# Spreading the slots' hidden inputs of six experts through a DRAM scratch tensor instead of TensorE products

## The chip, the cores and the metric

The kernel runs on one core of one Trainium2 chip. The metric is device time in microseconds (us), the median of several runs of the whole program. The engines are TensorE (PE, with its weight loads PEld), VectorE (DVE), ScalarE (ACT), GpSimd (POOL) and SyncE (SP, which here only issues DMAs).

## What is computed

Three layers in a row, in float32: an attention with a few global and some local keys (2 x 8 heads, 768 tokens, width 64), a soft mixture of experts over 32 slots, and a second mixture in which each of 1536 tokens goes to two of 8 experts. Cut to what matters here:

```python
# second layer; x is the soft layer's output, x = c @ slot_out: 32 slots' outputs mixed by the weights c
for e in range(E):                       # E = 8
    for k in range(2):
        mask = top2[:, k] == e
        h = np.maximum(x[mask] @ w1[e], 0.0)             # w1: 512 x 1024
        out[mask] += top2_w[mask, k, None] * (h @ w2[e]) # w2: 1024 x 512
```

The soft layer ends in a product with only 32 rows in the middle, so `x @ w1[e]` equals `c @ (slot_out @ w1[e])`. The kernel never makes x. It makes `g = slot_out @ w1[e]`, 32 x 1024, once for each expert, and then one product `c @ g` for each tile of 128 tokens.

## The kernel before, in words

The second layer is the stretch from 190 us to the end. Its work goes in tiles of 128 token rows, sorted by expert; each expert has at least two, here three or four, 28 in all. `run_tiles` calls `period(i, e, first, last)` for every tile i of every expert e, on each engine, with a first period, a loop over the middle ones and a last one. Each engine works through its own list in order.

A period on TensorE is: `down(0, i, e)`, twelve products of 512 columns with the first half of w2; `hidden` twice, eight products of 128 columns that make the next tile's h from `g_stack` (in the last period of an expert they read the next expert's part of it, and `wait_stack(e + 1)` stands before them); a transpose of a later tile's mixing weights; `down(1, i, e)`, twelve products with the second half. In the first period of an expert two things are added for the expert that follows, if `starts` says so (experts 2 to 7; experts 0 and 1 are made ahead of the loop): `slots_up(e + 1)` (line 1515) at its start makes g in bank 6, 128 partitions x 256 columns (four groups of 32 slots, one for each quarter of the 1024 columns), and `spread_slots_up(e + 1)` (line 1527) at its end lays it out as `g_stack` needs it.

g is kept as a sum of two float32r parts. ScalarE copies the high part to `g_hi` (`slots_up_high`), VectorE subtracts and stores the rest in `g_lo` (`slots_up_low`). `g_stack[:, e, :]` has 128 partitions x 1024: partitions 0 to 63 hold the high part twice, 64 to 127 the low part twice, and `c4T` holds the mixing weights split in the same way, so that one product over 128 partitions gives all the terms. Before the change eight products with the selection matrix `spread` (line 1538) put the parts in place in banks 2 and 3; ScalarE copies bank 2 and VectorE bank 3 to `g_stack` (`slots_up_spread`, lines 820 and 1141).

ScalarE also evacuates h (`hidden_high`, line 860) and the finished tile (`store_y`, line 880), and splits the next expert's w2 (`split_high`); VectorE makes the low parts (`hidden_low`, line 1224, `split_low`, line 1134). GpSimd fetches the mixing weights of a tile (line 667) and adds the stored tile to the output by an indirect DMA (line 695); it waits for the addition before it, and `store_y` waits for the addition of the tile two before, since `y_sb` has two buffers.

SyncE loads the weights, 2 MB for each of w1 and w2 of an expert, into a ring of four places, each from the fifth unit of this layer on in two halves of 1 MB with a wait for the first half before the second is issued. Its list `order` gives w1 and w2 by turns. Before it loads w1 of expert e + 2 it waits until `slots_up(e)` has used the place (`g_ready`), before w2 of e + 2 until w2 of e is split (`w_lo_stored`), and before w1 of expert 4 also until three tiles have been added to the output (`sums_before`, `out_added`).

Of the kernel before, what the change touches and what calls it, by code (L numbers as in the profile page):

```python
# [5 lines left out]
F32 = mybir.dt.float32  # L6
# [11 lines left out]
def attention_two_moe_layers(nc, q, k, v, n_global, n_local, phi, a_w1, a_w2,  # L18
# [52 lines left out]
    with ExitStack() as ctx:  # L71
# [214 lines left out]
        def sems(text):  # L286
            return [sem(n) for n in text.split()]
# [38 lines left out]
        tiles_ready, ids_made, hot_ready, slots_routed, tables_ready, rows_written = sems(  # L326
            "tiles_ready ids_made hot_ready slots_routed tables_ready rows_written")

        g_ready, g_hi_stored, g_lo_stored, g_spread, g_stored_act, g_stored_vec = sems(
            "g_ready g_hi_stored g_lo_stored g_spread g_stored_act g_stored_vec")  # L330
        w_hi_stored, w_lo_stored, w_rest_ready = sems("w_hi_stored w_lo_stored w_rest_ready")
        fetch_known, c_arrived, c4_ready, c4T_ready, c4T_stored = sems("fetch_known c_arrived c4_ready c4T_ready c4T_stored")
        first_arrived = [sem(f"first_arrived{n}") for n in range(FIRST)]
# [49 lines left out]

        ZERO_AFTER = (PAIRS - 1, NPAIR - 4)
        slot_rows = nc.dram_tensor("slot_rows", (N, ROW), F32).ap()
        block = ctx.enter_context(nc.Block())

        def path(eng):
# [41 lines left out]
        @block.sync  # L430
        def _(sp):
            def load_qk(p):
                b, hp = divmod(p, PAIRS)
                for n, t in enumerate((q, k)):
                    for h in range(2):
                        sp.dma_start(raw_qk[p % 2][n][:, :, h * HD:(h + 1) * HD],
                                     t[b, 2 * hp + h].rearrange("(i p) d -> p i d", p=P)).then_inc(qk_loaded[p % 2], 16)

            def load_v(p):
                b, hp = divmod(p, PAIRS)  # L440
                sp.dma_start(v_own[p % 2].rearrange("p h i d -> p (h i) d"),
                             v[b, 2 * hp:2 * hp + 2].rearrange("h (i p) d -> p (h i) d", p=P)).then_inc(v_loaded[p % 2], 16)

            def load_unit(n):
                layer, which, e = units[n]
                to, of = weights(units[n]), W[layer, which][e].rearrange("(c p) f -> p c f", p=P)
                chunks = to.shape[1] // halves(n)
                for h in range(halves(n)):
                    if h:

                        sp.wait_ge(unit_loaded[slot_of(n)], loaded(n) - 16)
                    own = slice(h * chunks, (h + 1) * chunks)
                    sp.dma_start(to[:, own], of[:, own]).then_inc(unit_loaded[slot_of(n)], 16)

            load_qk(0)
            load_qk(1)
            load_v(0)
            load_v(1)

            UNIT_AFTER = [p for p in range(-1, NPAIR - 2) if p != PAIRS - 1]  # L460
            assert len(UNIT_AFTER) == EARLY
            for p in range(-1, NPAIR - 2):
                if p + 3 < NPAIR:

                    sp.wait_ge(qk_transposed, 3 * (p + 2))
                    load_qk(p + 3)
                if p >= 0:

                    sp.wait_ge(heads_ready, QB * (p + 1))
                    load_v(p + 2)  # L470
                if p in UNIT_AFTER:
                    load_unit(UNIT_AFTER.index(p))
                if p in ZERO_AFTER:

                    sp.wait_ge(zeros_made, 1)
                    part = ZERO_AFTER.index(p)
                    first, end = [TT * n // len(ZERO_AFTER) for n in (part, part + 1)]
                    sp.dma_start(out.rearrange("(n p) d -> p n d", p=P)[:, first:end, :],
                                 zero_row[:].unsqueeze(1).to_broadcast([P, end - first, DM])).then_inc(rows_zeroed, 16)
                if p < 0:  # L480
                    sp.dma_start(phi_sb[:], phi.rearrange("(c p) s -> p c s", p=P)).then_inc(small_loaded, 16)
                    sp.dma_start(gate_sb[:, :, 0:E], w_gate.rearrange("(c p) e -> p c e", p=P)).then_inc(small_loaded, 16)
                    sp.dma_start(gate_sb[:, :, E:2 * E], w_noise.rearrange("(c p) e -> p c e", p=P)).then_inc(small_loaded, 16)

                    for t in range(TPG):
                        sp.dma_start(noise_sb[:, t * NG:(t + 1) * NG, :],
                                     noise.rearrange("(g t p) e -> t p g e", t=TPG, p=P)[t]).then_inc(small_loaded, 16)

            sp.wait_ge(heads_ready, UPB * B - QB)
            sp.wait_ge(qk_transposed, 3 * NPAIR)  # L490


            down1, up2, down2, up3, down3, up4 = range(2 * E + RING2 - 1, 2 * E + RING2 + 5)
            order = [*range(EARLY, down1), up2, down1, up3, down2, *range(down3, 4 * E)]
            sums_before = {down3: 1, up4: 3}
            for n in order:
                m = before_unit(n)
                if n == EARLY + 2:

                    sp.wait_ge(heads_ready, UPB * B)  # L500
                if n == EARLY + DURING:

                    sp.wait_ge(part_ready, 1)
                if n == up3:

                    sp.wait_ge(c4_ready, 1)
                if n in sums_before:

                    sp.wait_ge(out_added, ZEROED + 16 * sums_before[n])
                if m is not None:  # L510

                    layer, which, e = units[m]
                    if (layer, which) == (1, 2):
                        sp.wait_ge(w_lo_stored, FC * (e + 1))
                    else:
                        sp.wait_ge({(0, 1): hid_ready, (0, 2): soft_down_done, (1, 1): g_ready}[layer, which], e + 1)
                load_unit(n)


        @block.gpsimd  # L520
# [193 lines left out]
        def _(act):  # L714
# [98 lines left out]
            def slots_up_high(e):  # L813
                act.wait_ge(g_ready, e + 1)
                if e:

                    act.wait_ge(g_spread, e)
                copy(g_hi[:], bank[6][:, 0:FR]).then_inc(g_hi_stored, 1)

            def slots_up_spread(e):  # L820
                act.wait_ge(g_spread, e + 1)
                copy(g_stack[:, e, 0:F // 2], bank[2][:]).then_inc(g_stored_act, 1)
# [60 lines left out]
            def period(i, e, first, last):  # L883
                up_ahead, down_ahead = starts(e, first)
                if not (first and e == 0):
                    store_y(i, e - 1 if first else e)
                if up_ahead:
                    slots_up_high(e + 1)
                if not (last and e + 1 == E):
                    hidden_high(0, i + 1)  # L890
                if down_ahead:
                    wait_unit(act, (1, 2, e + 1))
                    for c in range(FC // 2):
                        split_high(e + 1, c)
                if not (last and e + 1 == E):
                    hidden_high(1, i + 1)
                if first and e == 0:
                    place_first(FIRST - 1)
                if up_ahead:
                    slots_up_spread(e + 1)  # L900
                if down_ahead:
                    for c in range(FC // 2, FC):
                        split_high(e + 1, c)

                if last and e + 1 == E:
                    store_y(i + 1, e)
# [6 lines left out]
        def _(dve):  # L913
# [222 lines left out]

            def slots_up_low(e):
                dve.wait_ge(g_hi_stored, e + 1)
                vec.tensor_tensor(g_lo[:], bank[6][:, 0:FR], g_hi[:], ALU.subtract).then_inc(g_lo_stored, 1)

            def slots_up_spread(e):
# [101 lines left out]
            def period(i, e, first, last):  # L1243
                up_ahead, down_ahead = starts(e, first)
                final = last and e + 1 == E
                if up_ahead:
                    slots_up_low(e + 1)
                if not final:
                    hidden_low(0, i + 1)
                    store_c4T(i + 2)  # L1250
                if down_ahead:
                    for c in range(FC // 2):
                        split_low(e + 1, c)
                if not final:
                    hidden_low(1, i + 1)
                if up_ahead:
                    slots_up_spread(e + 1)
                if down_ahead:
                    for c in range(FC // 2, FC):
                        split_low(e + 1, c)  # L1260
# [12 lines left out]
        def _(pe):  # L1273
# [328 lines left out]
                last.then_inc(y_ready if half else half_used, 1)  # L1602

            def wait_stack(e):
                pe.wait_ge(g_stored_act, e + 1)
                pe.wait_ge(g_stored_vec, e + 1)


            slots_up(1)
# [11 lines left out]
            def period(i, e, first, last):  # L1621
# [16 lines left out]
                        hidden(half, i + 1, e + 1 if last else e)  # L1638
                transpose_c4(i + 2)
                down(1, i, e)  # L1640
                if up_ahead:
                    spread_slots_up(e + 1)

            pe.wait_ge(tiles_ready, 1)
            run_tiles(pe, pe, period)

# [30 lines left out]
```

## Time and profile before

| what | value |
|---|---|
| time before, median of 3 runs | 403.64 us (402.04 to 405.11) |
| the profiled execution's own time | 402.48 us |
| its span from the first to the last instruction | 400.7 us |
| outside the span | 1.8 us |
| TensorE busy | 374.4 us (93% of the span) |
| VectorE, ScalarE, GpSimd busy | 200.8, 177.2, 219.3 us |
| HBM read, written | 77.88 MB, 11.19 MB |
| mean granted TensorE clock | 0.981 of full speed |

The profile is one execution. An engine's busy time counts overlapping instructions only once, but the duration printed for one matmul includes the part in which the next one already runs.

### The profile page before, as it was taken

Reading aid. Unit: us, or ns where it says so; the run is one execution under the profiler, and the core shown is the slowest. Engines: PE = TensorE matmul, PEld = TensorE weight load, DVE = VectorE, ACT = ScalarE, POOL = GpSimd, SP = SyncE. Lnnn points to the kernel's source line nnn. Section 1 sums busy time; section 2 is a strip of 40 time slices with the busy share of each in tenths; the row PEclk is TensorE's granted clock in tenths of the full one; section 3 lists DMA queues with packets and bytes.
Section 4 is the critical chain, followed back from the end, with each engine's and each line's share of the span. In section 5 each row is a group of like instructions: output and inputs, shape, how many; then the busy total and the mean of one; then the engine's idle time right before and its main releaser. Section 6 shows DMA issues by size and latency. Waiting matters only on the chain.

```text
span 400.7 us, 9118 instructions
## 1 busy us (share of the span) xinstructions
PE 374.4 (93%) x3084; PEld 281.7 (70%) x3084; DVE 200.8 (50%) x678; ACT 177.2 (44%) x441; POOL 219.3 (55%) x437
## 2 busy tenths in 40 slices
PE   6799999999988998889999999999999999999990
PEld 6466666666564666566887888878878878788870
DVE  2899988889452021382642625425426227254210
ACT  2676777776241100173633625435336237353310
POOL 3676776666601040234066747675676675756673
PEclk9999999999998999899999999999999999999995
DMA  8979899999999999993858778959768742422542
GB/s 162 249 191 306 215 249 268 288 324 319 391 402 339 389 395 397 391 388 125 291 166 239 184 241 250 239 146 216 219 126 243 224 78 31 56 35 30 61 52 34
DMA packets 73226, 89.62 MB, mean 224 GB/s; under 512 B 42768, under 2 KB 42816, under 8 KB 73184
## 3 DMA queue, kind: packets, MB, share of 16 engines
q1 hardware_dynamic: 67504, 79.85, 61.2%
q0 software_dynamic: 5392, 9.23, 15.5%
q8 instruction: 25, 0.41, 0.4%
q14 instruction: 17, 0.14, 0.1%
q10 hardware_dynamic: 288, 0.00, 0.0%
HBM read 77.88 MB, written 11.19 MB: 222 GB/s over the span
## 4 chain that ended last, share of the span: by engine, by line
PE 67%; DVE 15%; issue 14%; ACT 1%; DMA 1%; DVEq 1%; POOL 0%; ACTq 0%
PE y_bank L1598 25%; PE y_bank L1601 12%; PE bank L1589 6%; PE bank L1462 4%; PE y_bank L1495 4%; DVE arena L1028 4%; DVE row_sum L1036 3%; PE bank L1277 3%; PE bank L1523 3%; PE bank L1538 2%; PE bank L1547 2%; DVE row_inv L1050 2%; DVE arena L1044 1%; DMA counts_i<-in_n_local 1%; DVE neg_max L1028 1%
## 5 line engine op out<-in xcount | busy, mean ns | idle before, releaser
L1224 DVE SCALAR_TENSOR_TENSOR hT_lo<-bank,hT_hi 128x512 fp32r<-128x512 f32 x56 | 38.6, 691 | 104.7 <-ACT hT_hi L860 103.4
L1598 PE MATMUL y_bank<-w_hi,hT_hi 128*128 128x512 f32 x224 | 90.8, 405 | 0.2 <-ACT hT_hi L860 0.2
L1598 PE MATMUL y_bank<-w_lo,hT_hi 128*128 128x512 f32 x224 | 87.7, 392 | 0.0
L860 ACT ACTIVATE hT_hi<-bank 128x512 fp32r<-128x512 f32 x56 | 33.4, 598 | 102.0 <-PE y_bank L1601 60.5
L536 POOL TENSOR_TENSOR turn_mark<-turn_mark 128x1 f32<-128x1 f32 x140 | 41.7, 299 | 44.4 <-DMA out_rows<-arena,add_row 13.1
L599 POOL TENSOR_TENSOR arena<-arena,row_inv 128x512 f32<-128x512 f32 (+1 forms) x48 | 49.6, 1034 | 27.4 <-DVE row_inv L1050 25.3
L1601 PE MATMUL y_bank<-w_hi,hT_lo 128*128 128x512 f32 x224 | 60.2, 390 | 0.0
L767 ACT ACTIVATE arena<-arena,neg_max 128x256 f32<-128x256 f32 (+1 forms) x96 | 46.3, 483 | 25.1 <-DVE neg_max L1028 24.1
L695 POOL DMA_INDIRECT out_rows<-arena,add_row x28 | 45.1, 1609 | 15.4 <-issue 12.8
L1598 PEld LDWEIGHTS y_bank<-w_hi,hT_hi 128*128 128x128 f32 x224 | 42.7, 191 | 10.5 <-issue 2.8
L1601 PEld LDWEIGHTS y_bank<-w_hi,hT_lo 128*128 128x128 f32 x224 | 42.1, 188 | 9.4
L1598 PEld LDWEIGHTS y_bank<-w_lo,hT_hi 128*128 128x128 f32 x224 | 42.2, 188 | 7.7
L1028 DVE CUSTOM_DVE_ANT_0 arena<-bank,arena 128x256 f32<-128x256 f32 (+1 forms) x96 | 34.5, 396 | 9.6 <-issue 9.3
L667 POOL DMA_INDIRECT c_fetched<-slot_rows,fetch_row x28 | 31.4, 1122 | 14.2 <-issue 14.2
L1134 DVE TENSOR_TENSOR w_lo<-weight_ring,w_hi 128x512 fp32r<-128x512 f32 x56 | 35.3, 692 | 0.6
L1346 PE MATMUL bank<-arena 64*128 64x256 f32 (+1 forms) x192 | 33.1, 410 | 1.8 <-DVE neg_max L1028 0.9
L718 ACT ACTIVATE w_hi<-weight_ring 128x512 fp32r<-128x512 f32 x64 | 34.8, 620 | 0.0
L718 ACT ACTIVATE arena<-bank 128x512 f32<-128x512 f32 (+2 forms) x52 | 24.2, 490 | 20.2 <-PE bank L1277 8.2
L1277 PE MATMUL y_bank<-ident,arena 128*128 128x128 f32 x190 | 31.9, 287 | 0.7 <-POOL arena L599 0.4
L1044 DVE COPY arena<-y_bank 128x512 f32<-128x512 f32 (+1 forms) x48 | 30.5, 635 | 1.5 <-PE y_bank L1277 1.5
L1589 PEld LDWEIGHTS bank<-c4T,g_stack 128*128 128x128 f32 x224 | 29.2, 191 | 2.8 <-issue 0.7
L1277 PEld LDWEIGHTS y_bank<-ident,arena 128*128 128x128 f32 x190 | 19.9, 141 | 15.5 <-issue 10.1
(194 smaller groups left out, 563.4 us busy)
## 6 DMA issues: line engine op xcount, KB each, us to landing
weight_ring<-in_moe_w SPq DMA_DIRECT2D x16, 2048.0 KB, 11.9
weight_ring<-in_moe_w SPq DMA_DIRECT2D x22, 1024.0 KB, 5.7
arena<-in_moe_w SPq DMA_DIRECT2D x5, 2048.0 KB, 12.3
arena<-in_q SPq DMA_DIRECT2D x16, 192.0 KB, 6.0
arena<-in_k SPq DMA_DIRECT2D x16, 192.0 KB, 5.9
arena<-in_v SPq DMA_DIRECT2D x8, 384.0 KB, 4.9
out_rows<-zero_row SPq DMA_DIRECT2D x2, 1536.0 KB, 10.7
c_fetched<-slot_rows,fetch_row POOLq DMA_INDIRECT x28, 3.6
```

The lines of the kernel that those rows point to most:

```text
L536: g.tensor_tensor(turn_mark[:, turns[0]:turns[0] + 1], turn_mark[:, 0:1], turn_mark[:, 0:1], ALU.add)
L599: g.tensor_tensor(prob[u % 4][:, :, off:], prob[u % 4][:, :, off:], row_inv[:, u % 4, :].unsqueeze(2).to_broadcast([P, 2, WIN - off]), ALU ...
L695: pool.indirect_dma_start(out=out, out_offset=bass.IndirectOffsetOnAxis(ap=add_row[k][:, 0:1], axis=0), in_=y_sb[:, k], in_offset=None, bo ...
L718: return nc.scalar.activation(o, i, ACT.Copy)
L767: last = nc.scalar.activation(own, own, ACT.Exp, bias=neg_max[:, u % 2, h:h + 1], scale=-1.0, accum_out=row_sum[:, u % 4, h:h + 1])
L1028: vec.tensor_tensor_reduce(out=prob[u % 4][:, h, off:], in0=score_bank(u, h)[:, off:WIN], in1=bias8[:, 2 * pp + h, n0:n0 + nb], scale=-SCA ...
L1134: vec.tensor_tensor(w_lo[e % 2][:, c, :], weights((1, 2, e))[:, c, :], w_hi[e % 2][:, c, :], ALU.subtract).then_inc(w_lo_stored, 1)
L1224: vec.scalar_tensor_tensor(hT_lo[:, own, :].rearrange("p f t -> p (f t)"), bank[half][:], 0.0, hT_hi[:, own, :].rearrange("p f t -> p (f t ...
L1277: return nc.tensor.transpose(o, i, ident[:])
L1589: last = mm(bank[half][:, f * P:(f + 1) * P], g_stack[:, e, col:col + P], c4T[:], start=True, stop=True)
L1598: mm(y_of(i), hT_hi[:, n, :], w[e % 2][:, n, :], start=(n == 0 and w is w_hi), stop=False)
L1601: last = mm(y_of(i), hT_lo[:, n, :], w_hi[e % 2][:, n, :], start=False, stop=(n == FC - 1))
```

## The change

For experts 2 to 7 the products of `spread_slots_up`, and both copies of `slots_up_spread`, go. In their place SyncE writes `g_hi` and `g_lo` to a new DRAM tensor `g_rows`, waits until both are written, and issues four DMAs that read them into the four groups of 32 partitions of `g_stack`. For experts 2 to 5 this stands in SyncE's list directly before the load of w1 of expert e + 2, behind that load's other waits; for 6 and 7 behind the last load. `wait_stack` on TensorE waits for these reads (`g_stacked`). ScalarE and VectorE wait before they write `g_hi` and `g_lo` again until the earlier ones are in DRAM (`g_written`). Experts 0 and 1 stay as they were.

```diff
+        g_rows = nc.dram_tensor("g_rows", (E, 2, P, FR), F32).ap()
...
+            def stack_slots_up(e):
+
+                for k, stored in enumerate((g_hi_stored, g_lo_stored)):
+                    sp.wait_ge(stored, e + 1)
+                    sp.dma_start(g_rows[e, k], (g_hi, g_lo)[k][:].bitcast(F32)).then_inc(g_written, 16)
+                sp.wait_ge(g_written, 32 * (e - UP_EARLY + 1))
+                for k in range(4):
+                    sp.dma_start(g_stack[k * SLOTS:(k + 1) * SLOTS, e, :].bitcast(F32).rearrange("s (r f) -> s r f", r=NG),
+                                 g_rows[e, k // 2].rearrange("(r s) f -> s r f", r=NG)).then_inc(g_stacked, 16)
...
+                    if (layer, which) == (1, 1) and e >= UP_EARLY:
+                        stack_slots_up(e)
                 load_unit(n)
+            stack_slots_up(E - 2)
+            stack_slots_up(E - 1)
...
-                    act.wait_ge(g_spread, e)
+                    act.wait_ge(g_spread, min(e, UP_EARLY))
+                if e > UP_EARLY:
+
+                    act.wait_ge(g_written, 32 * (e - UP_EARLY))
                 copy(g_hi[:], bank[6][:, 0:FR]).then_inc(g_hi_stored, 1)
...
-                if up_ahead:
-                    slots_up_spread(e + 1)
...
             def slots_up_low(e):
                 dve.wait_ge(g_hi_stored, e + 1)
+                if e > UP_EARLY:
+
+                    dve.wait_ge(g_written, 32 * (e - UP_EARLY))
...
-                if up_ahead:
-                    slots_up_spread(e + 1)
...
             def wait_stack(e):
-                pe.wait_ge(g_stored_act, e + 1)
-                pe.wait_ge(g_stored_vec, e + 1)
+                pe.wait_ge(g_stored_act, min(e + 1, UP_EARLY))
+                pe.wait_ge(g_stored_vec, min(e + 1, UP_EARLY))
+                if e >= UP_EARLY:
+                    pe.wait_ge(g_stacked, 64 * (e - UP_EARLY + 1))
...
-                if up_ahead:
-                    spread_slots_up(e + 1)
-
```

## Rows read from the trace of the kernel before

**Rows 1.** The page: busy tenths of TensorE and its granted clock in 40 slices.

```profile
PE   6799999999988998889999999999999999999990
...
PEclk9999999999998999899999999999999999999995
```

**Rows 2.** Busy time by stretch, expert 1's periods.

```profile
217.40:239.90 22.50, 22.50 (x140) 18.25 (x139) 10.90 (x19) 10.45 (x19) 14.20 (x33) 1.00 0.76 229
```

**Rows 3.** Waits of TensorE from 190 to 400 us, all of them.

```profile
PE bank L1589 <- DVE c4T L1233: 0.5, 1, 0.5
PE y_bank L1598 <- ACT hT_hi L860: 0.2, 1, 0.2
```

**Rows 4.** The chain that ended last, in order of time: start, us, what.

```profile
217.52 1.86 PE bank L1523 x32
...
226.07 0.95 PE bank L1538 x8
227.02 1.85 PE y_bank L1598 x8
...
236.25 0.84 PE bank L1589 x8
...
326.74 1.86 PE bank L1523 x32
...
345.46 0.84 PE bank L1589 x8
...
386.19 7.64 issue
```

**Rows 5.** Line 1538: one of its two forms, duration ns min/median/max.

```profile
L1538 PE MATMUL bank<-g_hi,spread x32: 277/282/355, 174.3 to 358.3; 128*128 128x256 f32 x32
```

**Rows 6.** Timeline of ScalarE and VectorE in expert 1's first period.

```profile
227.06 0.60 ACT L718 ACTIVATE g_stack<-bank 128x512 fp32r<-128x512 f32 x1 [0.29 <-PE bank L1538]
...
219.87 0.42 DVE L1139 TENSOR_TENSOR g_lo<-bank,g_hi 128x256 fp32r<-128x256 f32 x1 [0.93 <-ACT g_hi L718]
...
227.54 0.67 DVE L1143 CAST g_stack<-bank 128x512 fp32r<-128x512 f32 x1
```

**Rows 7.** Timeline of SyncE's queue: half loads of 1 MB.

```profile
215.69 0.37 SPq L453 DMA_DIRECT2D weight_ring<-in_moe_w  x1
...
223.23 0.37 SPq L453 DMA_DIRECT2D weight_ring<-in_moe_w  x1
...
230.73 0.37 SPq L453 DMA_DIRECT2D weight_ring<-in_moe_w  x1
...
316.24 0.37 SPq L453 DMA_DIRECT2D weight_ring<-in_moe_w  x1
```

**Rows 8.** Waits of SyncE's queue from 190 to 400 us: total, times, longest.

```profile
SPq L453 <- PE bank L1523: 25.7, 3, 11.7
SPq L453 <- DVE w_lo L1134: 16.7, 4, 5.1
```

**Rows 9.** DMA issues: KB each, median us from issue to landing.

```profile
weight_ring<-in_moe_w SPq DMA_DIRECT2D x22, 1024.0 KB, 5.7
...
slot_rows<-arena POOLq DMA_DIRECT2D x3, 128.0 KB, 6.2
...
arena<-slot_rows,fetch_i POOLq DMA_INDIRECT x4, 2.6
noise_sb<-in_moe_noise SPq DMA_DIRECT2D x3, 16.0 KB, 4.7
```

**Rows 10.** GpSimd's additions to the output (line 695): timeline, then their landing; ScalarE's store of a tile.

```profile
231.16 1.59 POOL L695 DMA_INDIRECT out_rows<-arena,add_row  x1 [0.40 <-PE bank L1277]
...
339.61 0.37 POOL L536 TENSOR_TENSOR turn_mark<-turn_mark 128x1 f32<-128x1 f32 x1 [2.85 <-ACT arena L880]
...
DMA to landing us min/median/max: 4.7/4.9/8.4
...
240.57 0.68 ACT L880 ACTIVATE arena<-y_bank,arena  x1
```

More of the change, by code:

```diff
@@ L327, in attention_two_moe_layers @@
             "tiles_ready ids_made hot_ready slots_routed tables_ready rows_written")
-        g_ready, g_hi_stored, g_lo_stored, g_spread, g_stored_act, g_stored_vec = sems(
-            "g_ready g_hi_stored g_lo_stored g_spread g_stored_act g_stored_vec")
+        g_ready, g_hi_stored, g_lo_stored, g_spread, g_stored_act, g_stored_vec, g_written, g_stacked = sems(
+            "g_ready g_hi_stored g_lo_stored g_spread g_stored_act g_stored_vec g_written g_stacked")
         w_hi_stored, w_lo_stored, w_rest_ready = sems("w_hi_stored w_lo_stored w_rest_ready")
```

## The prediction, made before the changed kernel ran

> **What bounds the kernel now.** I read the page's slices first. TensorE stands at nine tenths and at full clock in nearly every slice [rows 1]. That alone doesn't say that it is the bound, since a matmul's busy time includes waiting inside the pipeline, so I went to the second layer, the only stretch that the change touches, and asked two questions. Is TensorE ever idle there? In expert 1's stretch it is busy for 22.50 of 22.50 us, at clock 1.00 [rows 2], and from 190 to 400 us it waited twice, 0.7 us in all [rows 3]. Does the end hang on it? The chain that ended last runs through TensorE without a break from expert 1 to the last tile's products, shortly before the "issue" piece at 386.19, and the eight products that the change removes are a link of it of their own, six times over, once for each expert from 2 to 7 [rows 4]. So in this stretch whatever TensorE no longer does is won in full, as long as nothing makes it wait instead; the whole question is whether a wait appears.
>
> **TensorE: the products.** Each expert from 2 to 7 loses the eight products of line 1538. Two rows give a price. By duration one takes 282 ns [rows 5], so eight would be 2.26 us and six experts 13.5 us. But durations overlap: in the chain the eight start at 226.07 and the next product starts at 227.02, which is 0.95 us [rows 4], or 119 ns from start to start. What TensorE gets back is the second number: 6 x 0.95 = 5.7 us. The same 0.95 stands before all six. The three engine waits in front of them (for both parts of g and the copies) were long satisfied; the one that `wait_stack` gains costs the sequencer an instruction in the last period, beside queued products, and I cost it at nothing.
>
> **ScalarE and VectorE: the copies.** Six copies of 0.60 us and six of 0.67 us go [rows 6]. Neither engine is the bound: in expert 1's 22.50 us they are busy 10.45 and 10.90 us [rows 2]. What the copies do is to push the eight-chunk splitting of w2 and the store of the finished tile back by their length and the wait for the products, 0.60 and 0.29 us on ScalarE [rows 6]. Once the products are gone the first period is 0.95 us shorter, and these two engines' lists shrink by 0.60 and 0.67 us and by the wait for the products, so their place relative to TensorE stays the same. Gain beyond TensorE's: none. The new waits on `g_written` before `g_hi` and `g_lo` are written again come a whole expert (over 20 us) after the writes they ask for, and are met unless the queue is late by that much. If one weren't, `hidden_high(0)` stands behind it on ScalarE and TensorE's next `down` behind that.
>
> **SyncE: what is added.** For each of six experts: two writes of 128 KB, a wait for both, four reads of 128 KB. Six issues at 0.37 us each [rows 7] are 2.2 us. The landings have no row of their own (SBUF to DRAM on this queue doesn't occur in the trace). The nearest rows: indirect fetches of a few hundred bytes a row land in 2.6 us, 16 KB on SyncE's queue in 4.7 us, a 128 KB store in short pieces from GpSimd in 6.2 us, and the slowest of the 28 additions to the output, 256 KB each beside weight loads, in 8.4 us [rows 9, 10]. Two landings in a row and the issues make the time c from g's parts being ready to `g_stack` being ready: from 2 x 2.6 + 2.2 = 7.4 us to 2 x 8.4 + 2.2 = 19.0 us, with 2 x 4.7 + 2.2 = 11.6 us by the row of SyncE's own queue and 14.6 us by the store. I take 11.6 us, as the same queue issued it; 128 KB instead of 16 adds little where 1 MB lands in 5.7 [rows 9].
>
> The Trainium skill ("DMA: Bandwidth & Descriptors", Anatomy of one DMA) gives some 2.0 us of fixed cost for a DMA, most of it the receipt of the last write, plus bytes over 436 GB/s. Its fit is for GpSimd's path; as an estimate from that page both writes would take 2.6 us and the four reads 3.2 us, and c would be 8.0 us. No row here shows such a DMA.
>
> **How long TensorE gives it.** `slots_up` ends at the start of the first period, and `wait_stack` comes in the last one, between `down(0)` and `hidden`. Expert 6's g, made in expert 5 with three tiles: products end at 328.60, 0.9 us later `g_lo` is stored (the 219.87 row with its 0.42, against 219.38 in the chain) [rows 6], so ready at 329.5; wanted at 345.46 less the 0.95 that goes in between, 344.5 [rows 4]: 15.0 us. Expert 7's g has the same pattern and the same 15.0 us. Experts with four tiles (2, 3 and 4, which make g for 3, 4 and 5) give one period of 6.5 us more. Expert 2's g has less: SyncE comes to it only behind the load's other wait, for three tiles added to the output, and in the trace issues there at 223.23 [rows 7], not at 220.3. Wanted at 236.25 - 0.95 = 235.3 [rows 4]: 12.1 us. With c = 11.6 all six are hidden, expert 2's by half a microsecond only. With 14.6 expert 2's alone comes 2.5 us late.
>
> **What is queued behind on SyncE.** The load of w1 of expert e + 2 starts later by the two writes (up to about 6 us) and four issues, and so do all later ones. SyncE now waits for TensorE and VectorE for 25.7 and 16.7 us in this stretch, up to 11.7 us at once [rows 8]: that is the slack which takes it up. Nothing needs the loads soon: w1 of expert 4 is issued at 223.23 [rows 7] and used in expert 3's first period, two experts of 22.5 us or more later [rows 2]. The last half load is issued at 316.24 [rows 7]; with some 6 us of writes and issues added before each w1 and the slack taken off, I expect it at about 320, landed at 326, and it is used no sooner than behind expert 5's last period, past 345.46 - 5 = 340 [rows 4]. A worse effect would be stacks that queue behind a load: expert 3's writes come behind w2 of expert 4. One half load is 5.7 us [rows 9], expert 3's budget is 21 us: 17.3 against it, hidden. TensorE's weights therefore cost nothing; were this cover gone, each late load would cost its lateness one to one at `slots_up` or the splits.
>
> **GpSimd.** Nothing is added to its list, but its additions share the DMA engines. It isn't far from being late: its addition issued at 231.16 takes the longest landing, 8.4 us, and ScalarE's store of the tile after next starts at 240.57, 1.0 us behind that landing [rows 10]. On the other side, in every late first period it waits for ScalarE (2.85 us at 339.61), and so catches up before the next expert; therefore the end of the kernel moves with TensorE.
>
> **The sum.** The profiled execution took 402.48 us, 400.7 of them the span. 402.48 - 5.7 = 396.8. That execution lies 1.16 us under the median of the runs, so against the median it is 403.64 - 5.7 = 397.9 us, 1.4% faster.
>
> **Rivals.**
> - Partly hidden: c is near the 128 KB store's 14.6 us. TensorE waits at `wait_stack` of expert 2, for 2.5 us; gain 3.2, time 400.4. For it: the tightest place has half a microsecond in my own sum. Against it: the store's pieces were short, these are 1 KB. Chance 0.14.
> - Slower: the round trip through DRAM is longer than the work between `slots_up` and `wait_stack` in the three-tile experts. The price is (c - 12.1) + 2(c - 15.0) for experts 2, 6 and 7, and it decides from the point where that is 5.7, c = 15.9 us. At the upper bound, c = 19.0, it is 14.9: 403.64 + 9.2 = 412.8 us. For it: writing and reading each have to be confirmed, beside fetches and additions. Against it: 1 MB on this queue lands in 5.7 us and both landings would need some 7. Chance 0.08.
> - GpSimd's additions land later because 0.77 MB more per expert pass the DMA engines. At the rate of the weight loads (1 MB in 5.7 us) that is up to 4.2 us once per expert; 1.0 us of it is covered by the margin above and about 2 us by ScalarE's own idle time before `hidden_high`. So 1.2 us each at most where it falls on the tight tile, which has happened once in six experts; taken for three of six it is 3.6, time 401.5. Chance 0.05. The Trainium skill says against this change that DMAs started from different engines run on the same 16 DMA engines and interleave ("DMA: Bandwidth & Descriptors", Issuing engines are not separate DMA queues); the trace agrees, in that the 8.4 us landing lies beside the load issued at 230.73.
> - The products' durations count in full: 13.5 us, time 390.1. Against it stands the chain. Chance 0.02.
> - That the change doesn't do what it says: banks 2 and 3 stand free, but nothing uses them; the text removes the products for all six. No chance of its own.
>
> **How the numbers follow.** The forecast has 0.71, the rivals 0.29. A measurement of this kernel can tell some 1% from no change, 4.0 us. The forecast's 5.7 lies above that with about 1 us to either side for the median's own scatter: some 0.66 of its 0.71 come out over 1%, and 0.02 of the last rival and a little of the others, 0.71 in all. Between: the rest of the forecast, the partly hidden case, GpSimd's and part of the third, 0.22. Slower by over 1%: 0.07. The range begins 2 us under the forecast, for scatter and a small extra gain, and reaches 402.0 so that it holds both partial cases; outside stay the slower case, the largest gain and the tails, under 0.2.
>
> **What would show each step right or wrong.** The chain should have no line 1538 after 190 us, and a first period of about 8.5 us from `slots_up` to the next tile's `down` in place of 9.5. TensorE's waits: none at `hidden` for a DMA on `g_stack`; one of up to 3 us in expert 1's last period is the second case, three or more the slower one. SyncE's queue: write to read issue in 4 to 6 us, reads down in about 5, the last load issued near 320 us. GpSimd's landings near 4.9 us in the median still. HBM written should rise by 1.6 MB and read by 3.1 MB. The prediction is wrong if TensorE waits, or if SyncE falls so far behind that weights come late.

## The result and the profile after

The changed kernel takes 407.92 us (405.17 to 412.67, 6 runs) against 403.69 us before: ratio 1.0115, 95% interval 1.0078 to 1.0153. It is 1.2% slower; 397.9 us had been forecast. Every ratio, here and below, compares the executions of the fast state alone, while a time in us is the median of all of them, so the two can differ by a few tenths of a per cent. The profiled execution took 405.17 us, 403.4 of them the span.

First, does TensorE still hardly ever wait? All its waits from 190 to 403 us, after:

```profile
PE bank L1294 <- POOL c L720: 7.5, 4, 3.2
PE y_bank L1615 <- ACT hT_hi L878: 0.2, 1, 0.2
```

Before, the only two were 0.7 us together [rows 3]. The new one isn't a wait for `g_stack`: none stands in this trace. Line 1294 is the transpose of a later tile's mixing weights, `transpose_c4`, and it waits for GpSimd's copy of the fetched weights into `c4`. So the stacks came in time and something else was late. Where in time? These are the six `slots_up`, from the timeline of TensorE after (start us, us):

```profile
216.40 1.93 PE L1540 MATMUL bank<-weight_ring,arena 128*32 128x256 f32 x32
237.86 1.93 PE L1540 MATMUL bank<-weight_ring,arena 128*32 128x256 f32 x32
270.65 1.93 PE L1540 MATMUL bank<-weight_ring,arena 128*32 128x256 f32 x32
298.58 1.93 PE L1540 MATMUL bank<-weight_ring,arena 128*32 128x256 f32 x32
331.46 1.93 PE L1540 MATMUL bank<-weight_ring,arena 128*32 128x256 f32 x32
353.00 1.93 PE L1540 MATMUL bank<-weight_ring,arena 128*32 128x256 f32 x32
```

Take the differences of the start times. Before, an expert with three tiles took 22.5 us [rows 2, 4] and one with four 6.5 us more, 28.9. Now experts 1, 3 and 5 take 21.5, 27.9 and 21.5 us: each has its 0.95 us less, as forecast. Expert 2 takes 32.8 and expert 4 32.9 in place of the 28.0 that the saving alone would leave: they lose 4.8 and 4.9 us. So the saving is 0.95 us in each of these five stretches, 4.8 in all, and the loss 9.7. The sixth saving falls behind the last of these rows: 9.7 - 5.7 = 4.0 us later in all, less 1.05 us by which this execution began the stretch earlier (216.40 against 217.45), is 2.95, and the profiled executions stand 2.7 us apart. What the loss in expert 4 looks like, from the timeline of TensorE after:

```profile
322.67 1.00 PE L1606 MATMUL bank<-c4T,g_stack 128*128 128x128 f32 x8
326.90 0.48 PE L1294 MATMUL bank<-ident,c 128*128 128x128 f32 x1 [3.23 <-POOL c L720]
327.03 0.78 PE L1615 MATMUL y_bank<-w_hi,hT_hi 128*128 128x512 f32 x1
327.61 0.63 PE L1615 MATMUL y_bank<-w_lo,hT_hi 128*128 128x512 f32 x1
```

TensorE stands for 3.2 us, and the eight products behind it take 0.63 us each in place of 0.39. The busy times of these stretches say why; the column before the last two is the granted clock:

```profile
319.00:322.60 3.60, 3.60 (x17) 2.97 (x16) 0.69 (x1) 0.60 (x1) 0.25 (x2) 1.00 0.92 241
...
327.00:330.40 3.40, 3.40 (x9) 2.72 (x10) 0.29 (x1) 0.00 (x0) 1.92 (x6) 0.52 0.98 311
```

The granted clock was 1.00 before the stall and 0.52 in the row behind it, about the lower of its two levels (1.2 in place of 2.4 GHz). In the chain the eight products take 3.24 us where they took 1.85, so 1.4 us come on top of the 3.2.

Expert 2 loses about as much in another way: three waits for the same copy, of 0.7, 2.1 and 1.5 us, the first at 250.77 us. TensorE is idle for 4.3 us of this stretch, and the clock stays at 1.00:

```profile
237.90:268.00 30.10, 25.80 (x154) 21.04 (x154) 11.52 (x21) 11.75 (x21) 16.52 (x39) 1.00 0.82 244
```

Why was GpSimd late? Its two waits for DMAs from 190 to 403 us, after (total, times, longest):

```profile
POOL turn_mark L551 <- DMA out_rows<-arena,add_row: 17.9, 9, 4.6
...
POOL turn_mark L551 <- DMA c_fetched<-slot_rows,fetch_row: 12.7, 6, 3.5
```

Before they were 13.1 us (13 times, 2.2 the longest) and 5.1 us (3 times, 2.1 the longest). The additions to the output land later, in the median after 5.4 us against 4.9 and at the worst after 9.3 against 8.4 [rows 10]. For the fetches of mixing weights the view after gives no landing; GpSimd's waits for them are the sign. GpSimd's list for one tile is serial: issue a fetch, wait for the addition before, issue the next addition, wait for the fetch, copy it into `c`. So either DMA, landing late, delays the copy for which TensorE waits.

In expert 4 it was the additions. From the chain that ended last, after (start, us, what):

```profile
305.04 8.43 DMA out_rows<-arena,add_row
314.41 9.34 DMA out_rows<-arena,add_row
324.69 1.59 POOL out_rows L710
326.90 0.48 PE bank L1294
```

The first was issued beside the four reads of expert 5's stack (304.30 to 306.04) and the half load behind them (306.09), the second beside two half loads issued together:

```profile
314.58 0.92 SPq L454 DMA_DIRECT2D weight_ring<-in_moe_w  x2
```

In expert 2 it was fetches. The first late one, seen beside SyncE's queue: first GpSimd's timeline after, then SyncE's.

```profile
235.32 1.11 POOL L682 DMA_INDIRECT c_fetched<-slot_rows,fetch_row  x1 [0.52 <-issue]
...
242.73 0.18 POOL L551 TENSOR_TENSOR turn_mark<-turn_mark 128x1 f32<-128x1 f32 x1 [3.47 <-DMA c_fetched<-slot_rows,fetch_row]
...
233.73 0.91 SPq L454 DMA_DIRECT2D weight_ring<-in_moe_w  x2
...
243.40 0.37 SPq L454 DMA_DIRECT2D weight_ring<-in_moe_w  x1
243.86 0.45 SPq L460 DMA_DIRECT2D g_rows<-g_hi  x1
244.36 0.43 SPq L460 DMA_DIRECT2D g_rows<-g_lo  x1
249.45 1.81 SPq L463 DMA_DIRECT2D g_stack<-g_rows  x4
```

A fetch of 128 short rows is issued at 235.32 and has landed at 242.7, 7.4 us later; the one issued at 235.94 in the kernel before landed in 3.9 us. In the same time SyncE has two half loads in flight, issued together at 233.73: the second half of w1 and the first of w2. The copy behind this fetch still comes in time, with 0.15 us to spare; the next three make TensorE wait. Of the fetches behind it, the one issued at 251.90, beside the reads of expert 3's stack and one half load, takes 7.0 us, and the one of 260.62, beside two half loads, 6.4 us. Before, the second half of w1 went out at 228.11 and w2's first at 230.73 [rows 7], since SyncE then waited for the splitting of w2; now it comes late, finds that wait long met and issues both at once. The same happens with each of the four units of w1, at 233.73, 258.62, 284.65 and 314.58 us. In a milder form it was there before: the half issued at 228.11 was in flight until 233.9, that of 230.73 went out beside it, and the addition issued at 231.16 was the one that took 8.4 us.

The stacks themselves are fairly quick. From the page after (KB each, median us to landing):

```profile
weight_ring<-in_moe_w SPq DMA_DIRECT2D x22, 1024.0 KB, 6.7
...
g_stack<-g_rows SPq DMA_DIRECT2D x24, 128.0 KB, 2.9
```

and from SyncE's timeline after, expert 2's:

```profile
221.91 0.34 SPq L460 DMA_DIRECT2D g_rows<-g_hi  x1
222.31 0.42 SPq L460 DMA_DIRECT2D g_rows<-g_lo  x1
```

Its reads are issued from 224.12 to 226.0 and the last of them lands 5.2 us after its issue at 225.47, so c is 221.91 to 230.7, 8.8 us. For the six experts it is 7.5 to 10.6 us, the longest for expert 3. The half loads now take 6.7 us in the median against 5.7 [rows 9].

### The profile page after: what moved, and what is told of

Same layout as the page of the kernel before. It is cut to its first block, busy times and chain, and to the rows that moved or that the text cites. A ratio compares the mean times of both kernels' runs of the same rounds, so it can differ in the third digit from the quotient of the medians.

```text
span 403.4 us, 9048 instructions
## 1 busy us (share of the span) xinstructions
PE 370.4 (92%) x3036; PEld 277.7 (69%) x3036; DVE 197.0 (49%) x672; ACT 173.5 (43%) x435; POOL 220.4 (55%) x437
## 4 chain that ended last, share of the span: by engine, by line
PE 31%; issue 25%; DVE 16%; DMA 13%; POOL 12%; POOLq 1%; ACT 1%; DVEq 1%; ACTq 0%
DMA out_rows<-arena,add_row 12%; PE y_bank L1615 8%; DVE arena L1044 4%; PE y_bank L1512 4%; PE y_bank L1618 4%; PE bank L1479 4%; DVE row_sum L1052 4%; POOL out_rows L710 3%; POOL c_fetched L682 3%; POOL turn_mark L551 3%; PE bank L1294 3%; DVE row_inv L1066 2%; PE bank L1606 2%; PE bank L1564 1%; DVE arena L946 1%
## 5 line engine op out<-in xcount | busy, mean ns | idle before, releaser
L1615 PE MATMUL y_bank<-w_hi,hT_hi 128*128 128x512 f32 x224 | 91.8, 410 | 0.2 <-ACT hT_hi L878 0.2
L1044 DVE CUSTOM_DVE_ANT_0 arena<-bank,arena 128x256 f32<-128x256 f32 (+1 forms) x96 | 34.5, 395 | 10.6 <-issue 10.3
## 6 DMA issues: line engine op xcount, KB each, us to landing
arena<-in_moe_w SPq DMA_DIRECT2D x5, 2048.0 KB, 12.1
```

The source lines that it names most:

```text
L1044: vec.tensor_tensor_reduce(out=prob[u % 4][:, h, off:], in0=score_bank(u, h)[:, off:WIN], in1=bias8[:, 2 * pp + h, n0:n0 + nb], scale=-SCA ...
L1615: mm(y_of(i), hT_hi[:, n, :], w[e % 2][:, n, :], start=(n == 0 and w is w_hi), stop=False)
```

## The experiments

Each time stands beside the kernel before on the same chip, which gave 403.2 to 403.7 us in the four groups of runs. Four theories are told apart: the saving of TensorE is not real because GpSimd's chain is the bound anyway (C); weight loads that SyncE issues late, and so two at a time, delay GpSimd's DMAs (A); the stacked transfers' own bytes delay them (B); `g_stack` comes late. Experiments 1, 2, 6, 7, 11, 13 and 14 leave out the stacks of experts 2 to 7 as an input: `hidden` reads those of experts 0 and 1, so TensorE's work stays whole and waits for no transfer.

**1. Is TensorE's saving real?** Kernel before without the products, nothing in their place.

```diff
-                if up_ahead:
-                    spread_slots_up(e + 1)
...
-  ... g_stack[:, e, col:col + P] ...
+  ... g_stack[:, e % UP_EARLY, col:col + P] ...
```

> The kernel before, without the products and copies of the spread for experts 2 to 7 and with nothing in their place: hidden reads the parts of g_stack of experts 0 and 1 in turn, so the rows of experts 2 to 7 are made from the wrong g. Theory A (GpSimd's DMAs land later because the weight loads behind the stacked transfers are pushed together) and theory B (they land later because of the stacked transfers' own bytes) both expect the whole of TensorE's saving, 6 x 0.95 = 5.7 us: about 398 us. Theory C (GpSimd's chain of fetch and addition is the bound already and swallows any saving of TensorE) expects 402 to 404 us.

Measured 397.70 us, ratio 0.9834 (0.9799 to 0.9870): 6.0 us less by the medians, 5.7 expected. Theory C falls. TensorE's waits are the two of before:

```profile
PE bank L1585 <- DVE c4T L1231: 0.5, 1, 0.5
PE y_bank L1594 <- ACT hT_hi L860: 0.2, 1, 0.2
```

**2. SyncE's delay without the bytes.**

```diff
-  sp.dma_start(g_rows[e, k], (g_hi, g_lo)[k][:].bitcast(F32))
+  sp.dma_start(g_rows[e, k, 0:16, 0:128], (g_hi, g_lo)[k][0:16, 0:128].bitcast(F32))
   # the four reads: 16 partitions x 128 columns each; no wait for g_stacked on TensorE
```

> The changed kernel, with SyncE's same sequence of two writes, wait and four reads, each cut to 16 partitions of 512 bytes, and with hidden reading experts 0's and 1's g_stack and not waiting for the reads (the rows of experts 2 to 7 are made from the wrong g). SyncE's delay stays nearly whole, 0.77 MB per expert go to 0.05. Theory A expects most of the loss to stay: 404 to 408 us. Theory B expects it to go: 398 to 400 us.

Measured 403.84 us, ratio 0.9997 (0.9967 to 1.0027): 6 us over the first, at next to no bytes, just under what A expected and well above what B did. TensorE waits for GpSimd's copy again, from 190 us on:

```profile
PE bank L1295 <- POOL c L720: 3.6, 3, 2.3
```

**3. The changed kernel with one load at a time.**

```diff
+                if n > down3:
+                    sp.wait_ge(unit_loaded[slot_of(n - 1)], loaded(n - 1))
                 load_unit(n)
```

> The changed kernel, with one more wait on SyncE: from w1 of expert 4 on, no unit's first half is issued before the second half of the unit before it has landed, so never more than 1 MB of weights is in flight. The stacked transfers stay. Theory A expects GpSimd's landings to fall back towards 5 us and the time to 399 to 403 us. Theory B expects no better than the changed kernel, 405 to 409 us, since SyncE only gets later.

Measured 405.39 us, ratio 1.0020 (0.9984 to 1.0056). The interval lies under that of the changed kernel, so the wait helps, but by 2 to 4 us only and not to 399 to 403: theory A's range is missed, and the median lies in B's. Neither theory alone. TensorE also waits once for a stack here:

```profile
PE bank L1608 <- DMA g_stack<-g_rows: 2.6, 1, 2.6
```

**4. The same transfers from ScalarE's queue.**

```diff
+                if up_ahead:
+                    write_slots_up(e + 1)   # behind hidden_high(0)
...
+                if up_ahead:
+                    read_slots_up(e + 1)    # behind hidden_high(1)
```

> The changed kernel, with the same writes and reads issued by ScalarE in the first period (writes behind hidden_high of the first half, reads behind that of the second), and SyncE's list as it was before the change. The bytes are the same, the weight loads are no longer pushed. Theory A expects the loss to go, 398 to 401 us, if ScalarE's six issues of about 0.4 us don't hold anything up. Theory B expects 405 us or more.

Measured 403.96 us, ratio 0.9980 (0.9947 to 1.0014). It lies between the two ranges and doesn't tell A from B, because the edit brought a stall of its own. ScalarE's timeline (an execution of 406.63 us): it waits for its writes, issues, and the tile's store behind that comes at 236.44.

```profile
232.27 2.02 ACTq L832 DMA_DIRECT2D g_stack<-g_rows  x4
234.34 2.19 ACT L719 ACTIVATE w_hi<-weight_ring 128x512 fp32r<-128x512 f32 x4 [4.27 <-issue]
236.44 0.67 ACT L895 ACTIVATE arena<-y_bank,arena  x1
```

**5. Writes from ScalarE where it is idle (directly behind `slots_up_high`), reads from SyncE between w1's halves.**

```diff
                         sp.wait_ge(unit_loaded[slot_of(n)], loaded(n) - 16)
+                        if (layer, which) == (1, 1) and e - 2 >= UP_EARLY:
+                            read_slots_up(e - 2)
```

> The changed kernel with its work split otherwise: ScalarE issues the two writes right behind slots_up_high, where it waits for TensorE anyway, and SyncE issues the four reads between the two halves of w1's load, where it waits anyway. All bytes stay; the loads are pushed by the four issues (1.5 us) and the reads only. Theory A (the pushed loads do the harm) expects 398 to 400 us, near the kernel without products. Theory B (the bytes do) expects 402 us or more. Both together, as the last runs suggest: about 401 us.

Measured 407.37 us, ratio 1.0096 (1.0058 to 1.0134), within B's open range and far from A's 398 to 400. SyncE's timeline (an execution of 414.10 us) shows why it doesn't separate the two all the same: the reads, w1's second half and w2's first go out in a row, from 230.18 to 232.9, 2.5 MB at once.

```profile
230.18 1.29 SPq L461 DMA_DIRECT2D g_stack<-g_rows  x3
231.51 0.43 SPq L461 DMA_DIRECT2D g_stack<-g_rows  x1
231.98 0.95 SPq L456 DMA_DIRECT2D weight_ring<-in_moe_w  x2
```

**6. Small transfers, one load at a time.** The edits of 2 and 3 together.

> The kernel with the small transfers (same sequence on SyncE, 0.05 MB per expert, hidden reads experts 0's and 1's g_stack), with one more wait: from w1 of expert 4 on no unit's first half is issued before the unit before it has landed. If the harm is that two half loads are in flight at once (theory A in its narrow form), 397 to 400 us. If it is only that the loads run later and without pauses, 402 to 405 us as without this wait.

Measured 398.29 us, ratio 0.9843 (0.9790 to 0.9895), where 2 alone had 0.9997: 0.0154, some 6 us with 2 to either side. The last half load is even issued later, at 331.9 against 326.0 us, but never two at once, and TensorE's one wait is

```profile
PE y_bank L1618 <- ACT hT_hi L880: 0.2, 1, 0.2
```

**7. The opposite: loads of 2 MB, SyncE never late.** The kernel of 1 with

```diff
-            return 2 if n > 2 * E + RING2 else 1
+            return 1
```

> The kernel without products (nothing in their place, hidden reads experts 0's and 1's g_stack), with every unit loaded as one transfer of 2 MB instead of two halves with a wait: SyncE is never late, but 2 MB are in flight at once each time. Theory A in its narrow form expects it 4 us or more slower than with halves: 402 us or more against 397.7. If two halves in flight don't matter, 397 to 399 us.

Measured 410.50 us, ratio 1.0183 (1.0133 to 1.0233), 12.8 us over the kernel of 1 (14 by the ratios), with no stack in it at all. GpSimd's waits for additions and fetches and TensorE's for it:

```profile
POOL turn_mark L536 <- DMA out_rows<-arena,add_row: 17.1, 7, 4.7
...
POOL turn_mark L536 <- DMA c_fetched<-slot_rows,fetch_row: 14.1, 5, 3.8
...
PE bank L1273 <- POOL c L705: 7.8, 6, 2.5
```

These are the changed kernel's rows over again. With 6 this shows theory A in its narrow form: more than one half load in flight does harm. It doesn't show that nothing else does.

What counts in GpSimd's waits is not their sum. In experiment 6 it waits 18.7 us for fetches, more than in the changed kernel, and nothing is lost; but there the longest single wait for a DMA is 2.6 us, against 4.6 in the changed kernel and 4.7 here. Short waits fit into the time that each copy into `c` has to spare: in the kernel before, from 200 to 356 us, the copies ended 1.5 to 6.4 us ahead of the transposes that read them. One of the tightest, from the timelines of GpSimd and TensorE before:

```profile
256.96 0.79 POOL L705 COPY c<-c_fetched 128x128 f32<-128x128 f32 x1
...
259.38 0.29 PE L1277 MATMUL bank<-ident,c 128*128 128x128 f32 x1
```

**8. Kernel 5 with one load at a time** (the edit of 3).

> The kernel with ScalarE's writes and SyncE's reads between the halves, with the wait that leaves never more than one half load in flight. Theory A: as good or up to 2 us better than without this wait, 397 to 400 us. Theory B: no better than 402 us.

Measured 402.55 us, ratio 0.9961 (0.9926 to 0.9996), against 1.0096 without the wait. The wait is worth some 5 us, but A's 397 to 400 us is missed and B's "no better than 402" came out. This is the lowest ratio of a version of the whole computation, 1.6 us under the kernel before and so within 1% of it; it can't be told from experiments 4, 10 and 15.

**9, 10. Reads landed before the next load,** in kernels 3 and 8.

```diff
+                sp.wait_ge(g_stacked, 64 * (e - UP_EARLY + 1))
```

> The changed kernel with one load at a time and, in addition, SyncE waits until the four reads of a stack have landed before it issues the next load. All bytes stay. If what hurts GpSimd's DMAs is the amount in flight at once (1 MB of weights plus 0.5 MB of reads behind SyncE's back), this gives 399 to 402 us against 405.4 without the wait. If it is the stacked transfers' bytes or their short pieces as such, 404 to 407 us; a stack of a three-tile expert that comes late would cost 1 to 3 us of that, and would show as TensorE waiting for g_stack.

> ScalarE's writes, SyncE's reads between the halves, one load at a time, and in addition the reads must have landed before the second half is issued. In flight theory: 398 to 400 us against 402.6 without that wait. Bytes as such: 402 to 404 us.

Measured 410.18 us, ratio 1.0165 (1.0117 to 1.0214), and 403.06 us, ratio 0.9974 (0.9941 to 1.0007). Neither gained. The first is over both of its expected ranges, the second in that of the bytes. In the first TensorE waits for a stack once, for 5.7 us, together with GpSimd's lateness (in the second also once, 3.3 us); that SyncE's chain has become too long is the likely reason, and no run tests it.

```profile
PE bank L1609 <- DMA g_stack<-g_rows: 5.7, 1, 5.7
PE bank L1297 <- POOL c L723: 3.4, 6, 1.0
```

**11. Whole writes, small reads, one load at a time.** Kernel 6 with the writes of 128 KB back.

> Small transfers and one load at a time (398.3 us), but with the two writes to DRAM whole, 128 KB each; only the reads stay small, and hidden reads experts 0's and 1's g_stack. If the reads are what costs the rest: 398 to 400 us. If the writes to DRAM are: 402 to 405 us.

Measured 399.46 us, ratio 0.9847 (0.9783 to 0.9912), not to be told from kernel 6: the writes cost nothing that can be seen, with some 3 us to either side.

**12. The kernel before with one load at a time.**

> The kernel before with one load at a time, nothing else changed. TensorE waited 0.7 us in all in the second layer of the kernel before, so no theory expects a gain of more than 1 us: 402 to 404 us. A gain of 3 us or more would say that the loads' grouping alone, and not its meeting with the change, is worth that.

Measured 404.08 us, ratio 1.0005 (0.9968 to 1.0042). As expected, the wait is worth nothing that can be seen there; TensorE's waits are the two of before, 0.7 us.

**13, 14. TensorE doesn't wait for the stacks:** kernel 3 and the changed kernel, all bytes kept, `hidden` reading experts 0's and 1's `g_stack`.

> The changed kernel with one load at a time and all the bytes of the stacks, but hidden reads experts 0's and 1's g_stack and TensorE doesn't wait for the reads. With the wait it took 405.4 us and TensorE waited once for g_stack, with small transfers 398.3. If what is left with one load at a time is mainly g_stack that comes late, this gives 398 to 401 us. If it is the bytes beside GpSimd's DMAs, 403 to 406 us.

> The changed kernel with nothing on SyncE changed; only hidden reads experts 0's and 1's g_stack and TensorE doesn't wait for the reads. The trace of the changed kernel shows no wait of TensorE for g_stack, so no gain is expected if the loss runs over GpSimd alone: 406 to 409 us. If hidden waits for g_stack matter in most executions: 403 us or less.

Measured 404.33 us, ratio 1.0017 (0.9985 to 1.0049), and 408.14 us, ratio 1.0087 (1.0049 to 1.0126). Neither can be told from its pair with the wait (1.0020 and 1.0115), so lateness of `g_stack` isn't the main cause in either; up to some 3 us of it would not show. And 13 against 11 leaves the reads' bytes (3.1 MB in 24 reads, in pieces of 1 KB) with 1.0017 - 0.9847 = 0.017, about 7 us, with 3 to either side.

**15. Writes from ScalarE, reads ahead of w1, one load at a time.**

> A version of the whole computation: writes issued by ScalarE right behind slots_up_high, reads by SyncE before the load of w1 and so behind the load still in flight, one load at a time. SyncE no longer waits for its own writes, g_stack comes earlier than with the writes on SyncE, and the reads run beside the tail of a load instead of ahead of a new one. If lateness of g_stack is what is left: 399 to 401 us, the best full version. If the bytes are: 402 to 404 us.

Measured 403.53 us, ratio 0.9978 (0.9942 to 1.0014): the case "bytes". GpSimd's longest wait for an addition is 3.9 us, TensorE's for GpSimd 1.2.

## Why the prediction was wrong

The forecast let the transfers cost TensorE nothing. Measured, they cost some 11 us: the changed kernel's ratio is 1.0115, that of the kernel without products and without transfers 0.9834. The steps that failed are the last half of "What is queued behind on SyncE" and "GpSimd". Point by point, by the prediction's own steps:

- **TensorE's saving** was right: 0.95 us by start times and not 2.26 by durations, six times. The undisturbed experts after are 0.95 us shorter, and the kernel of experiment 1 gained 6.0 us.
- **ScalarE and VectorE** at nothing: right as far as seen; the new waits on `g_written` appear in no list.
- **The round trip c** was put at 11.6 us and was 7.5 to 10.6; the 128 KB store from GpSimd and the 16 KB row were both too dear as neighbours. The estimate from the Trainium skill's "DMA: Bandwidth & Descriptors", Anatomy of one DMA (2.0 us and bytes over 436 GB/s, 8.0 us in all) was nearer for five of the six experts; the trace agrees with it within 1.7 us there, and expert 3's is 2.6 us longer. TensorE never waited for a stack in the profiled execution, so the budgets of 12.1 and 15.0 us held.
- **What is queued behind on SyncE** is the first step that failed. It asked only who needs the loads, found that nobody does soon, and set their lateness at nothing. The last half load went out at 325.01 (316.24 before, [rows 7]; about 320 forecast), and indeed no load came late to its user. But a late queue loses its pauses: half loads that SyncE's wait for VectorE had kept 2.6 us apart or more went out 0.44 us apart. Experiments 2 and 6 put a price on just this: 403.84 against 398.29 us.
- **GpSimd** is the second. The rival was there and named the right engine, but it was sized at 3.6 us and 401.5 us in total. It counted the stack's bytes once per expert against the additions, and followed a late addition only to ScalarE's store, with 1.0 us of margin [rows 10] and 2 us of ScalarE's idle time for which it shows no row. It left out the paired loads, and the other path: from a late addition or a late fetch through GpSimd's own list to the copy into `c`, for which TensorE waits directly at `transpose_c4`. The 4.3 and 3.2 us of waiting came on that path. It also left out what a stall can cost behind it: 1.4 us at half clock after the one of 3.2 us, nothing seen after those of 0.7 to 2.1. The sum as it was: a saving of 4.8 us by the last `slots_up`, a loss of 9.7.
- **"Slower: the round trip is longer than the work"** did not happen in the changed kernel, though the time did rise. A wait for a stack appears only with one load at a time, in experiments 3, 9 and 10 (2.6, 5.7 and 3.3 us, once each).

What was shown and what is left: that the loss runs through GpSimd's DMAs (the wait rows, 7 and 14), that pairs of half loads do harm (2 against 6, 1 against 7), and that the reads have a share of their own (11 against 13, with one load at a time). What each is worth depends on the order in which they are added, each step with 2 to 3 us to either side. Pairs first: 6 us with small transfers (2 against 6), then the bytes 3.6 us on top of them (14 against 2: 1.0087 - 0.9997). Bytes first: 7 us for the reads (13 against 11), then the pairs 3 us on top (14 against 13: 1.0087 - 1.0017). Either way it is some 10 us. Why 3.1 MB of reads cost so much stays open: their pieces of 1 KB, and that they fall on 32 partitions each, weren't varied.

The Trainium skill's rule that was weighed against this change ("DMA: Bandwidth & Descriptors", Issuing engines are not separate DMA queues: transfers started by different engines share the DMA engines and interleave) is what the trace shows: a fetch on GpSimd's queue took 7.4 us beside two half loads on SyncE's, and in experiment 7 up to 7.7. The prediction had this rule for its rival; the size was the point, and for that it had too small a number.

## What to carry to other kernels

When work is put on a queue, ask not only who needs what comes behind it, but what its waits had kept apart: a queue that falls behind issues in bursts, and here such bursts delayed the short transfers of another queue. Follow each engine that issues short DMAs to the one that waits for it, with the margin of each link in microseconds, before moving bytes from an engine to the DMA queues. Judge its waits by the longest one against that margin, not by their sum. A saving on the bounding engine that is bought with DMA traffic should be measured in two halves, the saving with nothing in its place and the traffic with nothing saved; here these were -6.0 us and about +10 by the medians.

## What the runs showed of the hardware

- A fetch of 128 rows of 288 bytes took 2.6 to 6.1 us in the kernel before (median 3.6). In the changed kernel one took 7.4 us with 2 MB of loads in flight, and an addition 9.3 us (median 4.9 before). Loading in transfers of 2 MB in place of 1 MB with a wait between cost 12.8 us (experiment 7 against 1), though the bytes and SyncE's order are the same.
- Writing 128 KB from SBUF to DRAM and waiting for it took 2.2 us on SyncE's queue for expert 2, from the first of two writes to the first read, and 5.6 us for expert 3, whose writes went out 0.5 us behind a half load. The reads, 128 KB in pieces of 1 KB, landed in 2.2 to 5.2 us.
- Behind 3.2 us without work the granted clock was 0.52 in the row from 327.0 to 330.4 us, and eight products of 512 columns took 3.24 us in place of 1.85. Behind waits of 0.7, 2.1 and 1.5 us it stayed at 1.00.
